# An attention kernel whose GpSimd operations for v, q and k and the weights are put at different tiles of a head

## The reference, cut to what matters

```python
scores = scale * np.matmul(q, k.transpose(0, 1, 3, 2))
thresh = np.max(scores, axis=-1, keepdims=True) - tau
scores = np.where(scores >= thresh, scores, -1000000000.0)
scores = scores - np.max(scores, axis=-1, keepdims=True)
attn = np.exp(scores)
attn = attn / (np.sum(attn, axis=-1, keepdims=True) + 1e-09)
return np.matmul(attn, v)
...
x = _moe_ref(x=x, **moe_kwargs)
return _moe2_ref(x=x, **moe2_kwargs)
```

## Time and profile before

| | |
|---|---|
| median of 3 runs | 1315.62 us (1315.33 to 1317.46) |
| profiled execution: its time | 1315.53 us |
| profiled execution: span | 1313.8 us |
| mean granted TensorE clock | 0.986 |
| attention | from the start to about 365 us |

### The profile page before, as it was taken

The page is one execution under the profiler, slowest core; times in us unless marked ns, Lnnn a source line. Parts: engine busy times, 40 slices in busy tenths (PEclk is TensorE's granted clock), DMA queues, the critical chain, the costliest instruction groups (busy, mean ns, idle before and its releaser), DMA issues.

```text
span 1313.8 us, 20231 instructions
## 1 busy us (share of the span) xinstructions
PE 1244.9 (95%) x7678; PEld 1135.9 (86%) x7678; DVE 622.8 (47%) x1249; ACT 539.4 (41%) x966; POOL 568.8 (43%) x412
## 2 busy tenths in 40 slices
PE   5999999999885999999999999998999999999998
PEld 4899999989864889989999999997999999999997
DVE  7888888888745521212212121215544535444433
ACT  5777787878742243333333333333212112112111
POOL 5989999989810344343524434454511101000000
PEclk9999999999986999999999999999999999999999
DMA  5545454453520143343424333344221102000000
GB/s 174 129 120 139 125 148 125 128 135 100 168 52 25 57 153 111 130 129 96 132 93 144 101 123 125 105 161 128 82 73 49 32 1 73 16 0 24 16 1 25
DMA packets 71170, 123.14 MB, mean 94 GB/s; under 512 B 11824, under 2 KB 30512, under 8 KB 71088
## 3 DMA queue, kind: packets, MB, share of 16 engines
q1 hardware_dynamic: 57216, 86.90, 23.4%
q0 software_dynamic: 6080, 19.93, 4.9%
q10 hardware_dynamic: 7792, 15.21, 3.1%
HBM read 82.43 MB, written 19.92 MB: 78 GB/s over the span
## 4 chain that ended last, share of the span: by engine, by line
PE 79%; POOL 6%; issue 5%; ACT 4%; DVE 3%; DMA 2%; SPq 0%; ACTq 0%; POOLq 0%
PE h_ps L702 32%; PE y_ps L721 11%; PE y_ps L720 11%; PE y_ps L719 11%; PE o_acc L560 5%; POOL probs_lo L1311 4%; PE ring L530 2%; PE ring L531 2%; PE t_ps L680 2%; PE ring L544 2%; PE ring L543 2%; POOL k_parts L1316 1%; DMA k_parts<-k_ones 1%; ACT q_hi L805 1%; ACT probs_hi L797 1%
## 5 line engine op out<-in xcount | busy, mean ns | idle before, releaser
L702 PE MATMUL h_ps<-x_hi,region_a 128*128 128x384 f32 (+1 forms) x1408 | 343.8, 317 | 4.8 <-DVE x_lo L1203 4.3
L702 PEld LDWEIGHTS h_ps<-x_hi,region_a 128*128 128x128 f32 x1408 | 246.5, 189 | 11.6 <-DVE x_lo L1203 5.2
L1311 POOL TENSOR_TENSOR probs_lo<-probs,probs_hi 128x576 fp32r<-128x576 f32 x160 | 226.6, 1427 | 34.0 <-ACT probs_hi L797 34.0
L702 PE MATMUL h_ps<-x_lo,region_a 128*128 128x384 f32 (+1 forms) x704 | 221.2, 314 | 0.0
L1213 DVE SCALAR_TENSOR_TENSOR h_lo<-h_ps,h_hi 128x256 fp32r<-128x256 f32 (+1 forms) x128 | 62.8, 491 | 311.6 <-ACT h_hi L896 288.4
L899 ACT ACTIVATE h_hi<-act_out 128x384 fp32r<-128x384 f32 (+1 forms) x112 | 53.7, 480 | 312.3 <-DVE act_out L1224 305.8
L719 PE MATMUL y_ps<-region_b,h_hi 128*128 128x512 f32 x448 | 175.7, 392 | 1.4 <-DVE h_lo L1230 1.4
L720 PE MATMUL y_ps<-region_b,h_hi 128*128 128x512 f32 x448 | 176.5, 394 | 0.0
L721 PE MATMUL y_ps<-region_b,h_lo 128*128 128x512 f32 x448 | 176.5, 394 | 0.0
L1297 POOL TENSOR_TENSOR region_b<-stage,region_b 128x1024 fp32r<-128x1024 f32 x40 | 95.8, 2399 | 143.5 <-ACT region_b L778 143.4
L896 ACT ACTIVATE h_hi<-h_ps 128x256 fp32r<-128x256 f32 (+1 forms) x128 | 56.0, 437 | 240.2 <-PE h_ps L702 231.9
(11 more groups left out here) (202 smaller groups left out, 2406.3 us busy)
## 6 DMA issues: line engine op xcount, KB each, us to landing
stage<-in_moe_w SPq DMA_DIRECT2D x56, 512.0 KB
qk_raw<-in_qk SPq DMA_DIRECT2D x32, 320.0 KB, 3.4
expert_rows<-rows_out ACTq DMA_DIRECT2D x8, 768.0 KB, 3.9
v_nat<-in_v SPq DMA_DIRECT2D x16, 320.0 KB, 3.6
k_ones<-q_hi SPq DMA_DIRECT2D x30, 160.0 KB, 2.6
q_lo<-k_parts SPq DMA_DIRECT2D x30, 160.0 KB, 2.4
q_hi<-q_hi SPq DMA_DIRECT2D x30, 160.0 KB, 2.4
k_parts<-k_ones SPq DMA_DIRECT2D x30, 160.0 KB, 2.9
```

The costliest lines, as they stand in the source:

```text
L702: mm = pe.matmul(h_ps[:, c % 2, 0:width], wt, x[kind][:, cc, :], start=(n == 0), stop=(n == 3 * C - 1))
L1311: pool.tensor_tensor(probs_lo[:, m % 4, :], probs[:, m % 4, :], probs_hi[:, m % 4, :].bitcast(F32), ALU.subtract).then_inc(lo_done, 1)
```

## The change

The change edits two things. `SPLIT_AT` puts the last eight weight splits every 15 slots instead of every 17. In GpSimd's program `v_lo` of head h is issued at the end of slot j = 4 of head h-1 instead of at the start of slot j = 0 of head h. `LOAD_W_AT` is not touched.

```diff
         LOAD_W_AT = {10: 4, 44: 5, 78: 6, 112: 7}
         SPLIT_AT = {-14: ((0, 0), (0, 1)), -9: ((1, 0), (1, 1)), -3: ((2, 0), (2, 1)), 2: ((3, 0),), 3: ((3, 1),)}
-        SPLIT_AT.update({22 + 17 * n: ((4 + n // 2, n % 2),) for n in range(8)})
+        SPLIT_AT.update({(4 + 3 * n) * NT + 2: ((4 + n // 2, n % 2),) for n in range(8)})
...
             def slot(i, c):
                 j = c % NT
-                if j == 0 and has(i, c // NT, NH, U):
-                    h = c // NT
-                    pair, lane = h % U // 2, h % 2
-                    wait(pool, v_hi_done, head(i, h) + 1)
-                    pool.tensor_tensor(v_lo[:, lane, :, 0:D], v_nat[:, pair, lane, :, :],
-                                       v_hi[:, lane, :, 0:D].bitcast(F32), ALU.subtract).then_inc(v_split, 1)
                 if has(i, c - 1, TILES, SL):
                     m = c - 1
                     wait(pool, hi_done, tile(i, m) + 1)
                     pool.tensor_tensor(probs_lo[:, m % 4, :], probs[:, m % 4, :], probs_hi[:, m % 4, :].bitcast(F32),
                                        ALU.subtract).then_inc(lo_done, 1)
+                if j == 4 and has(i, c // NT + 1, NH, U):
+                    h = c // NT + 1
+                    pair, lane = h % U // 2, h % 2
+                    wait(pool, v_hi_done, head(i, h) + 1)
+                    pool.tensor_tensor(v_lo[:, lane, :, 0:D], v_nat[:, pair, lane, :, :],
+                                       v_hi[:, lane, :, 0:D].bitcast(F32), ALU.subtract).then_inc(v_split, 1)
```

## The result

The changed kernel takes 1320.3 us (median of 6 runs, 1318.23 to 1321.93) against 1315.45 us before (median of 6): the ratio is 1.0036, with a 95% interval of 1.0023 to 1.0049. It is 4.85 us slower, and the interval is that of 3.0 to 6.4 us. The forecast was 1321.3 us, 5.8 us slower.

What follows compares the result with a forecast made beforehand. TensorE, busy 95% of the span, was taken to bound the kernel. Moved splits -0.4, the wait in slot 112 +3.9 and the clock +2.3 gave +5.8 us on 1315.53, so 1321.3 us, range 1318.0 to 1324.0.

Steps and rivals of the forecast that it cites:

- The likeliest case: ScalarE waits for piece 7's load in slot 112 and the clock falls: +5.8 us, 1321.3 us, chance 0.72.
- The place: Slot 112: ScalarE's high part waits 6.0 us for piece 7's load; TensorE restarts 5.7 us late, net +3.9 us.
- The first shadow: Slot 112: GpSimd's weight split falls within TensorE's pause, so its 0.80 us is not paid.
- The second: Next head: the 1.30 us wait for copies at 271.71 vanishes, since TensorE comes 5 us later.
- The clock: From slot 113: the pause drops TensorE to half speed for 5.2 us, costing 2.3 us.
- stall, but the clock holds: Rival at slot 112: a 5.7 us pause without a clock fall, +3.5 us, 1319.0 us, chance 0.15.
- Stall and clock together: Around slots 112 and 113: TensorE's 5.7 us late restart plus 2.3 us for the lowered clock.
- The six moved splits: Slots 37, 52, 67, 82, 97 and 127, now at j = 2: 0.78 us each, 4.68 in all.
- The copies: 0.46 us from slot 73's stretch, kept because removing its split need not bring the copies in time.
- A slip in a bound: Upper bound for the six moved splits: at 1.36 us each, 3.5 us is lost.
- The faster rival: Splits at j = 2 nearly free through GpSimd's idle time; without a stall 1310.0 us, chance 0.03.
- moves as a whole: Code behind attention is a chain on its result and shifts by attention's change, with no term of its own.

Runs made afterwards that it cites:

- the kernel in which it stayed up: Changed kernel with TensorE computing the scores of tile 122 twelve times in slot 114 to fill the pause: 1321.22 us, ratio 1.0037.
- load alone: Kernel before with only the load of piece 7 moved from slot 112 to slot 104: 1314.92 us, ratio 0.9992.
- j = 3: Changed kernel with all eight weight splits at j = 3 and the loads of pieces 6 and 7 in slots 74 and 104: 1311.08 us, ratio 0.9966.

## Why the prediction was right

The likeliest case came about, by its own steps. The measured 4.85 us and the forecast 5.8 can't be told apart, since the interval goes from 3.0 to 6.4.

- **The place.** "It waits for both transfers: 6.0 us in which ScalarE does nothing": 5.70 measured. "5.7 us" for TensorE's restart: a gap of 5.41. The first shadow held: 5.70 of waiting and 2.1 of clock are 7.8 of the head's 7.85, so GpSimd's split in slot 112 adds nothing to be seen. The second came true, the head behind took 10.30, but the stall is not shown to be the reason: the copies landed 2.8 us after their issue and not 4.3 as before, and the two kernels with the load in slots 104 and 109, which have no stall, take 10.29 for the same head. That this one split is the cause, and all of it, is shown by the kernel with one split moved and by the two with an earlier load.
- **The clock.** "2.3 us": 2.1, read against the kernel in which it stayed up (1.4 in the kernel with one split moved). The rival "stall, but the clock holds" is excluded by the windows.
- **Stall and clock together** were 8.0 us in the forecast and are 7.85 in the profile.
- **The six moved splits.** 0.78 each in the forecast, 0.77 to 0.80 in the profile.
- **The copies** were set at 0.46 and cost about 0.9 (0.85 of it at the head behind slot 76, with a gap of 1.1 us). This term was too small, so the six places brought no gain of 0.4 us. Their cause was wrong in part as well: the wait at 271.71 was put down to the load ahead of the copies, and 0.5 us of the two heads' 1.03 remained when that load was moved. The reading of 0.84 at 101.96 as a wait for copies, though the row names VectorE, is borne out by other runs: in seven of them the row at this place names the copies, with 0.9 to 1.5 us. It takes 0.56 of the 1.36 us booked for slot 39's split, which leaves 0.80, as for slot 124.
- **v_lo** costs nothing: 0.9999.
- **A slip in a bound.** With 1.36 for each of the six splits and 0.46 for the copies the sum is 8.62 against 5.54 before: 3.1 us lost, not 3.5. Nothing else rests on it.
- **The faster rival** ("the splits at j = 2 are nearly free") is false for j = 2, but the mechanism exists one tile further on. I had its price in hand, 0.46 for slot 73 with the copies in it, and did not ask why it was the smallest. The comparison of ready and used times above could have been made from the trace of before, and would have told that j = 3 is cheap. In that trace nearly all of the 0.46 is the wait for the copies:

```profile
186.78 0.37 PE L530 MATMUL ring<-k_parts,q_hi 128*128 128x288 f32 x1 [0.43 <-DMA k_parts<-k_ones]
```

- **What came behind attention "moves as a whole"** is the step that does not hold to a microsecond. From the start to `q_hi` of slot 26 the profile of after has 0.9 us more (81.21 against 80.34; the profiles of the study have 80.2 to 81.7 there). From there to the last `o_t` it has 5.9 more (283.45 before, 289.35 after). From there to the first matmul of the expert layer it is 54.4 us before and 51.5 after, in code that is the same, and behind that another 1.3 less. Together that is the 2.6 us between the two spans. So these two profiles agree with the forecast for attention, and show that code behind it can take back 4 us; they say nothing on the distance between 5.8 and 4.85, which is one of medians.

## What to carry to other kernels

Before moving a consumer in a table of slots, look up where its producer stands in the other tables. A load and its first use in the same slot cost the waiting engine the whole landing time, plus the time by which the issuing queue runs behind it, and hold up all that is queued behind. Here that was 5.7 us (3.2 of landing, 2.5 of lag) plus 2.1 us of clock; three slots of distance cost nothing, in one run. To place extra work on an engine that is nearly full, list for each of its results when it is ready and when it is used, and put the work ahead of the result with the most to spare, not where the list looks even.

## What the runs showed of the hardware

After a pause the granted clock fell from 2.4 to 1.2 GHz at about 269.96 us in the changed kernel, TensorE having stood still since 266.5, and it was back at about 276.8, TensorE having been busy since 271.9. In the kernel before it fell 2.6 us after the last matmul of attention's follow-up, and in the kernel with one split moved 2.0 us after the last matmul ahead of the stall. So the same pause is priced a little differently each time, 2.1 and 1.4 us in the two kernels with the stall.

The stretch from the last `o_t` to the first expert matmul is uneven too: 54.4 us (before), 51.5 (after), 53.1 (load in slot 104), 52.2 (load alone) and 53.6 (j = 3), with the same instructions in all. Between before and after the two traces show where the 2.9 us arise. About half of it, 1.5 us, is there 26 us behind `o_t`, and in this part TensorE has the lower clock for longer. Before, it fell at about 365.3 and came back at 375.6:

```profile
365.00:366.00 1.00, 0.08 (x2) 0.00 (x0) 0.81 (x3) 0.00 (x0) 0.00 (x0) 0.66 0.00 0
...
375.00:376.00 1.00, 1.00 (x9) 0.93 (x8) 0.00 (x0) 0.57 (x2) 0.00 (x0) 0.72 1.02 418
```

After, it fell at about 372.4 and came back at 379.2:

```profile
372.00:373.00 1.00, 0.14 (x1) 0.15 (x2) 0.73 (x3) 0.00 (x0) 0.14 (x1) 0.68 0.00 0
...
379.00:380.00 1.00, 1.00 (x8) 0.74 (x7) 0.00 (x0) 0.46 (x1) 0.00 (x0) 0.90 0.78 137
```

That is 10.2 us at the lower level against 6.8. Most of the other half, 1.1 us, is a wait for gathered rows at its end, whose last transfer GpSimd issued at 410.45 before and at 415.76 after. Before:

```profile
415.64 1.12 PE L680 MATMUL h_ps<-ident,rows_in 128*128 128x128 f32 x4 [1.52 <-DMA rows_in<-x_rows,idx_first]
```

After:

```profile
419.88 0.77 PE L680 MATMUL h_ps<-ident,rows_in 128*128 128x128 f32 x4 [0.45 <-DMA rows_in<-x_rows,idx_first]
```

The last 0.3 us are these transposes and what follows, at 1.2 GHz before and partly at 2.4 after. In the kernel before the clock came back at 423.3, five microseconds into the expert layer; in the changed kernel at about 420.2, before its first matmul at 422.1. That can bear on the 1.3 us behind that matmul, not on the stretch ahead of it. None of this was tried by itself.

The load of piece 7 landed 3.0 to 3.8 us after the issue of each of its transfers in all profiles but those in which TensorE repeated matmuls meanwhile, where its second transfer took 5.0 and 5.1. I had not expected it, and its cause is open.
